# Causal attention with decay, then two expert layers, on one Trainium2 core: single fp32 score products, with new load order, start and last pair

## What is computed

```
scores = q @ k.T / sqrt(64);  cum = cumsum(log(clip(f, 1e-4, 1)))
attn   = softmax(where(j > i, -1e9, scores + cum[i] - cum[j]))
x      = (attn @ v), heads side by side: [1152, 512]
logits = x @ w_gate; expert = argmax; gate = its softmax probability
expert layer: relu(x @ w1[e]) @ w2[e], at most 288 rows an expert, times gate
dense layer:  h = x @ w_in; g = h if h >= 1, 0 if h <= -1, else (h+1)^2/4; out = g @ w_out
```

## Time and profile before

| | |
|---|---|
| median of 3 runs | 605.24 us (604.88 to 606.43) |
| the profiled execution | 605.88 us |
| its span, first to last instruction | 604.0 us |
| TensorE busy | 574.3 us (95%) |
| weight loads | 511.4 us (85%) |
| VectorE busy | 334.3 us (55%) |
| ScalarE busy | 286.5 us (47%) |
| GpSimd busy | 62.7 us (10%) |
| mean granted TensorE clock | 0.990 |

### The profile page before, as it was taken

How to read it: one execution, slowest core, us unless ns; L and a number is a source line. 1 busy time by engine, 2 the same in 40 slices (tenths; PEclk the granted TensorE clock), 3 DMA queues, 4 the chain that set the end, 5 groups by cost and what they waited for, 6 DMA issues and landing times.

```text
span 604.0 us, 9717 instructions
## 1 busy us (share of the span) xinstructions
PE 574.3 (95%) x3774; PEld 511.4 (85%) x3774; DVE 334.3 (55%) x657; ACT 286.5 (47%) x570; POOL 62.7 (10%) x75
## 2 busy tenths in 40 slices
PE   7869999999999999999999999989999999999993
PEld 3658888878448999999999999989999999999992
DVE  3748888875703545658456584786443543453432
ACT  3647777774303444736446364575333333333330
POOL 8301111110250500000000000000000200010001
PEclk9979999999999999999999999999999999999998
DMA  6984755520154056254562645633000100000001
GB/s 135 288 187 117 186 121 119 150 71 0 43 179 166 25 186 209 74 206 148 195 212 76 208 145 173 240 106 105 1 0 1 53 0 2 1 18 36 0 1 52
DMA packets 52973, 63.95 MB, mean 106 GB/s; under 512 B 31136, under 2 KB 31136, under 8 KB 52928
## 3 DMA queue, kind: packets, MB, share of 16 engines
q1 hardware_dynamic: 50960, 58.56, 32.0%
q0 software_dynamic: 1968, 4.77, 2.2%
HBM read 58.55 MB, written 4.77 MB: 105 GB/s over the span
## 4 chain that ended last, share of the span: by engine, by line
PE 81%; DVE 5%; SPq 4%; issue 3%; DMA 2%; POOL 2%; ACT 2%; DVEq 0%; ACTq 0%
PE ps L652 11%; PE ps L653 11%; PE ps L654 11%; PE ps L726 5%; PE ps L727 5%; PE ps L728 5%; PE ps L709 5%; PE ps L711 5%; PE ps L710 5%; PE ps L535 4%; PE ps L497 3%; PE ps L516 2%; PE ps L550 2%; POOL x_scratch L423 1%; SPq L313 1%
## 5 line engine op out<-in xcount | busy, mean ns | idle before, releaser
L276 DVE TENSOR_TENSOR slot<-stage,slot 128x1024 fp32r<-128x1024 f32 x80 | 95.4, 1221 | 20.7 <-ACT slot L269 20.7
L269 ACT ACTIVATE slot<-stage 128x1024 fp32r<-128x1024 f32 x80 | 81.4, 1052 | 4.6 <-DMA stage<-in_moe_w_in_dram 2.6
L872 ACT ACTIVATE act_t<-ps,half 128x384 f32<-128x384 f32 x48 | 27.9, 582 | 115.2 <-PE ps L711 115.2
L1138 DVE SCALAR_TENSOR_TENSOR act_t<-act_t 128x384 f32<-128x384 f32 x48 | 26.8, 558 | 99.1 <-ACT act_t L872 99.1
L652 PE MATMUL ps<-xe,slot 128*128 128x288 f32 x256 | 75.8, 296 | 0.3 <-DVE xe L1090 0.3
L653 PE MATMUL ps<-xe,slot 128*128 128x288 f32 x256 | 75.6, 295 | 0.0
L653 PE MATMUL ps<-hid,slot 128*128 128x288 f32 x256 | 75.6, 295 | 0.0
L654 PE MATMUL ps<-xe,slot 128*128 128x288 f32 x256 | 75.3, 294 | 0.0
L654 PE MATMUL ps<-hid,slot 128*128 128x288 f32 x256 | 75.3, 294 | 0.0
L652 PE MATMUL ps<-hid,slot 128*128 128x288 f32 x256 | 75.2, 294 | 0.0
L847 ACT ACTIVATE hid<-ps 128x288 fp32r<-128x288 f32 x64 | 26.5, 415 | 99.6 <-PE ps L654 98.7
(11 more groups left out here) (147 smaller groups left out, 1073.0 us busy)
## 6 DMA issues: line engine op xcount, KB each, us to landing
stage<-in_moe_w_dram SPq DMA_DIRECT2D x32, 1024.0 KB, 5.2
cb<-c_scratch SPq DMA_DIRECT2D x16, 288.0 KB, 3.6
x_sorted<-x_scratch SPq DMA_DIRECT2D x9, 258.0 KB, 4.8
cb<-c_scratch SPq DMA_DIRECT2D x16, 144.0 KB, 4.3
q_nat<-in_q_dram SPq DMA_DIRECT2D x16, 128.0 KB, 3.6
k_nat<-in_k_dram SPq DMA_DIRECT2D x16, 128.0 KB, 2.6
v_nat<-in_v_dram SPq DMA_DIRECT2D x16, 128.0 KB, 4.1
stage<-in_moe_w_in_dram SPq DMA_DIRECT2D x2, 1024.0 KB, 6.1
```

The lines of the kernel that those rows point to most:

```text
L269: nc.scalar.activation(s[:, 0, at], stages[n_buf][:, at], ACT.Copy).then_inc(w_hi, 1)
L276: nc.vector.tensor_tensor(s[:, 1, at], stages[stage_of(g)[0]][:, at], s[:, 0, at].bitcast(F32), ALU.subtract).then_inc(w_lo, 1)
```

## The change

- **Scores.** `q_t` and `k_t` hold one fp32 value; `qk_low` and the low parts are gone. `score` makes one fp32 product a head and tile where there were three fp32r ones.
- **Loads.** The first pair's keys, the decay inputs of its two heads and of all heads are issued by ScalarE. SyncE loads pairs 0, 1 and 2 and v of pair 0 before it waits for the decay sums; a pair's q and k are loaded two pairs ahead, pair 3 between weight chunks 0 and 1.
- **Decay sums.** Those of pair 0 are made on all partitions at once (spread load of f, logarithm, two scans), without the way through DRAM. The scan for the other heads comes after the first row maxima. `fl` lies in `xl`.
- **Weight parts.** High parts of the six halves at steps 6, 11, ... 31, low parts at 11, 16, ... 36, after the splitting of the probabilities.
- **128-row forms.** `ot` has 640 columns, the last 64 zero, so that the last tile's product with the router's weights has the full form; a matrix `shift` does the same for the row sums.
- **Start.** q and k of pair 0 are transposed into two banks (6 and 2) without a wait between.
- **Last pair.** The second product with v is cut into the tiles that need only the low parts up to the last but one (banks 0 and 1) and the last tile (bank 6). The logits of the earlier heads are summed ahead of time (`lg`), those of the last two are added.

```diff
+        q_t = sb("q_t", [P, 2, QT], F32, att)
+        k_t = sb("k_t", [P, 2, S], F32, att)
...
+        ot = sb("ot", [P, 2, NT * P], F32, att)
...
+        fl = xl[0:BH].rearrange("p h t c -> p (h t c)")[:, 0:3 * S].rearrange("p (r s) -> p r s", r=3)
...
-        EARLY = {n: (i // 2, i % 2) for i, n in enumerate([9, 14, 19, 24, 29, 34])}
+        EARLY_HI = {NT * (i + 1) + 1: (i // 2, i % 2) for i in range(6)}
+        EARLY_LO = {NT * (i + 2) + 1: (i // 2, i % 2) for i in range(6)}
...
-            load_pair(0)
-            sp.wait_ge(f_steps, 3)
-            sp.dma_start(c_dram[:, :], fl[:, 0, :]).then_inc(c_out, 16)
-            sp.wait_ge(c_out, 16)
-
...
+                if p >= 1:
+                    load_keys(sp, p)
+
+            def load_decay(p):
                 if p >= 2:
                     sp.wait_ge(maxed, UNITS * (p - 1))
-                    sp.wait_ge(v_lo, p - 1)
-                for hh in range(2):
-                    sp.dma_start(cb[:, p % 2, hh, :], c_dram[2 * p + hh:2 * p + hh + 1, :].partition_broadcast(P)
-                                 ).then_inc(c_in[p % 2], 16)
+                sp.dma_start(cb[:, p % 2, 0:2, :], c_dram[2 * p:2 * p + 2, :].partition_broadcast(P)).then_inc(c_in[p % 2], 16)
                 for hh in range(2):
                     sp.dma_start(cb[64 * hh:64 * hh + 64, p % 2, 2, :],
                                  c_dram[2 * p + hh:2 * p + hh + 1, :].partition_broadcast(64)).then_inc(c_in[p % 2], 16)
-                if p == 0:
...
+            def load_v(p):
+                b, h = divmod(2 * p, HEADS)
+                if p >= 2:
+                    sp.wait_ge(v_lo, p - 1)
...
-            load_decay_and_v(0)
-            load_decay_and_v(1)
+            load_pair(0)
+            load_pair(1)
+            load_v(0)
+            load_pair(2)
+            sp.wait_ge(f_steps, 3)
+            sp.dma_start(c_dram[:, :], fl[:, 0, :]).then_inc(c_out, 16)
+            load_v(1)
+            sp.wait_ge(c_out, 16)
+            load_decay(1)
             load_chunk(sp, 0)
+            load_pair(3)
             load_chunk(sp, 1)
             load_chunk(sp, 2)
             for p in range(2, PAIRS):
-                load_pair(p)
-                load_decay_and_v(p)
+                load_decay(p)
+                load_v(p)
+                if p + 2 < PAIRS:
+                    load_pair(p + 2)
                 if p == 4:
                     load_chunk(sp, 3)
...
+        def qk_bank(p, j):
+
+            return 2 if p == 0 and j == 1 else 6
...
             def score(n):
                 p, t = divmod(n, NT)
                 if t == 0:
-                    pe.wait_ge(qk_lo, 2 * p + 2)
+                    pe.wait_ge(qk_sb, 2 * p + 2)
                 if n >= 1:
                     pe.wait_ge(maxed, units_to(n - 1))
                 qs = slice(Q0[t], Q0[t] + P)
-                parts = ((0, 0), (1, 0), (0, 1))
                 if t < LAST:
-                    for i, (a, b) in enumerate(parts):
-                        for hd in range(2):
-                            r = slice(64 * hd, 64 * hd + 64)
-                            mm(bank(hd, W[t]), q_t[r, p % 2, a, qs], k_t[r, p % 2, b, 0:W[t]], start=(i == 0), stop=False)
+                    for hd in range(2):
+                        r = slice(64 * hd, 64 * hd + 64)
+                        mm(bank(hd, W[t]), q_t[r, p % 2, qs], k_t[r, p % 2, 0:W[t]], start=True, stop=False)
                     for hd in range(2):
                         last = mm(bank(hd, P, Q0[t]), ident_b[:], mask_b[:], start=False, stop=True)
                 else:
-                    for i, (a, b) in enumerate(parts):
-                        mm(bank(0), q_t[:, p % 2, a, qs], k_t[:, p % 2, b, 0:Q0[t]], start=(i == 0), stop=(i == 2))
-                        mm(bank(1, D), q_t[:, p % 2, a, qs], k_t[:, p % 2, b, Q0[t]:S], start=(i == 0), stop=False)
+                    mm(bank(0), q_t[:, p % 2, qs], k_t[:, p % 2, 0:Q0[t]], start=True, stop=True)
+                    mm(bank(1, D), q_t[:, p % 2, qs], k_t[:, p % 2, Q0[t]:S], start=True, stop=False)
                     last = mm(bank(1, D), ident_b[:], mask4_b[:], start=False, stop=True)
                 last.then_inc(scores, 1)
...
+            def output_tile(p, hd, t, to):
+
+                return mm(to, ot[:, hd, P * t:P * t + P], rg[:, (2 * p + hd) % HEADS, :], start=True, stop=True)
+
             def output(p, hd, b):
 
                 if p == 0 and hd == 0:
-                    pe.wait_ge(wg_in, 16 * 2 * HEADS)
+                    pe.wait_ge(wg_in, 32)
                     pe.wait_ge(consts, 1)
                 if hd == 0:
                     pe.wait_ge(exped, UNITS * (p + 1))
-                    mm(bank(b, 1, 448, 64), ident[:, 64:128], rowsum[:, p % 2, 0, LAST:NT], start=True, stop=True).then_inc(sum_ps, 1)
+                    mm(bank(b, 1, 448), shift[:], rowsum[:, p % 2, 0, LAST:NT], start=True, stop=True).then_inc(sum_ps, 1)
                 pe.wait_ge(o1_sb, 2 * p + hd + 1)
                 pe.wait_ge(o2_sb, 2 * p + hd + 1)
                 for t in range(NT):
-                    last = mm(bank(b, XC, XC * t, QN[t]), ot[:, hd, Q0[t]:W[t]], rg[:, (2 * p + hd) % HEADS, :], start=True, stop=True)
+                    last = output_tile(p, hd, t, bank(b, XC, XC * t))
                 last.then_inc(ox_ps, 1)
...
-            spin(6, 2)
-            pe.wait_ge(qk_lo, 1)
             transposed(0, 1)
-            spin(6, 2)
+            spin(8, 4)
             score(0)
...
+            pe.wait_ge(pt_lo, UNITS * PAIRS - 1)
+            pe.wait_ge(maxed, UNITS * PAIRS)
+            times_v_full_tiles(0, 0)
+            times_v_full_tiles(1, 1)
+            pe.wait_ge(exped, UNITS * PAIRS)
+            mm(bank(2, 1, 448), shift[:], rowsum[:, end % 2, 0, LAST:NT], start=True, stop=True).then_inc(sum_ps, 1)
+            for hd in range(2):
+                pe.wait_ge(o1_sb, 2 * end + hd + 1)
+                for t in range(2):
+                    output_tile(end, hd, t, bank(5 + 2 * hd, XC, XC * t))
+            pe.wait_ge(pt_lo, UNITS * PAIRS)
             pe.wait_ge(xl_sb, 2 * end)
-            times_v_second(end, 1, 6)
-            spin(4, 0)
-            pe.wait_ge(o1_sb, 2 * end + 2)
-            output(end, 0, 7)
-            output(end, 1, 6)
+            for hd in range(2):
+                times_v_last_tile(hd, 6, D * hd)
+            for hd in range(2):
+                pe.wait_ge(o2_sb, 2 * end + hd + 1)
+                for t in range(2, LAST):
+                    last = output_tile(end, hd, t, bank(5 + 2 * hd, XC, XC * t))
+                last.then_inc(ox_ps, 1)
+            pe.wait_ge(o_last, 1)
+            pe.wait_ge(r_inv, 3 * PAIRS)
+            for hd in range(2):
+                last = output_tile(end, hd, LAST, bank(2, XC, XC * hd))
+            last.then_inc(ox_last, 1)
...
+            act.dma_start(cb[:, 0, 0:2, :], f[0, 0:2, :].partition_broadcast(P)).then_inc(f0_in, 16)
+            load_keys(act, 0)
+            act.dma_start(fl[:, 0, :], f.rearrange("b h s -> (b h) s")).then_inc(f_in, 16)
+            act.wait_ge(f0_min, 1)
+            A.activation(ot[:, :, 0:S], cb[:, 0, 0:2, :], ACT.Ln).then_inc(f0_log, 1)
+            act.wait_ge(f_steps, 2)
...
+                if n in EARLY_HI:
+                    cut_hi(*EARLY_HI[n])
...
+            dve.wait_ge(f0_in, 16)
+            V.tensor_scalar(cb[:, 0, 0:2, :], cb[:, 0, 0:2, :], 1.0e-4, 1.0, ALU.max, ALU.min).then_inc(f0_min, 1)
             dve.wait_ge(f_in, 16)
             V.tensor_scalar(fl[:, 0, :], fl[:, 0, :], 1.0e-4, 1.0, ALU.max, ALU.min).then_inc(f_steps, 1)
-            V.memset(fl[:, 2, :], 1.0).then_inc(f_steps, 1)
-            dve.wait_ge(f_log, 1)
             dve.wait_ge(f_steps, 2)
-            V.tensor_tensor_scan(fl[:, 0, :], fl[:, 2, :], fl[:, 1, :], 0.0, ALU.mult, ALU.add).then_inc(f_steps, 1)
+            dve.wait_ge(f0_log, 1)
+            for hd in range(2):
+                V.tensor_tensor_scan(cb[:, 0, hd, :], ones, ot[:, hd, 0:S], 0.0, ALU.mult, ALU.add).then_inc(f0_sum, 1)
...
-            def qk_low(p, j):
-                dve.wait_ge(qk_hi, 2 * p + j + 1)
-                if j == 0:
-                    V.scalar_tensor_tensor(out=q_t[:, p % 2, 1], in0=bank(6, QT), scalar=-float(D) ** -0.5,
-                                           in1=q_t[:, p % 2, 0].bitcast(F32), op0=ALU.mult, op1=ALU.subtract).then_inc(qk_lo, 1)
-                else:
-                    V.tensor_tensor(k_t[:, p % 2, 1], bank(6, S), k_t[:, p % 2, 0].bitcast(F32), ALU.subtract).then_inc(qk_lo, 1)
-
...
+            dve.wait_ge(f_log, 1)
+            V.tensor_tensor_scan(fl[:, 0, :], ones[0:BH], fl[:, 1, :], 0.0, ALU.mult, ALU.add).then_inc(f_steps, 1)
...
+                if n in EARLY_LO:
+                    cut_lo(*EARLY_LO[n])
+                if n == 32:
+                    V.tensor_reduce(lg[:, 0:NT, :], xl[:, 0:HEADS, :, D:XC].rearrange("p h t e -> p t e h"), AX_X, ALU.add
```

(37 more changed lines are left out.)

120 lines of the change are left out of this document (57 added, 63 removed).

## The result

The changed kernel takes 588.51 us (median of 4 runs, 588.12 to 589.55); the kernel before, measured beside it, 605.06 (604.66 to 606.43). The ratio is 0.9725, with a 95% interval of 0.9705 to 0.9745: 16.5 us faster. The forecast was 595.0 with a range of 587 to 604, so the range held the time, near its low end, and rival A had the size. The profiled execution took 588.54 us, 17.34 less than that of before.

What follows compares the result with a forecast made beforehand. TensorE was taken as nearly full in all but the first slices. From the profiled 605.88: +2.8 (later pairs), -6.4 (stall), -3.7 (start), -3.0 (last pair) gave 595.6; the median, 0.64 lower, 595.0 us; range 587 to 604.

Steps and rivals of the forecast that it cites:

- rival A: Half-row fp32 score products: both heads overlap fully, 1.05 us a pair less than forecast, 587 us; chance 0.15.
- Score products: TensorE's score groups: one fp32 product a head instead of three fp32r ones adds 1.55 us a pair.
- three slots: Score group's four records: head 0's first, its second beside head 1's first, head 1's second; 2 passes each, 6N columns.
- 4N: Columns a score group streams with both heads fully overlapped, N being the tile's columns; +0.5 us a pair.
- k-low wait: TensorE's wait for VectorE's low part of k goes when qk_low is dropped: -0.15 us a pair.
- Weight cuts: VectorE's low cut moved from ahead of the 256-column maxima: -0.57 us a pair, -1.11 in the last.
- 128-row forms: Output and row-sum products of the last tile avoid switching to the 64-column form: -0.3 us a pair.
- Stall: Pair 0 to pair 1: loading pair 2 ahead of the weight chunks removes stall and slow clock; -6.4 us net.
- Start: Up to pair 0's last-tile scores: first scores at 10.4 instead of 13.09, last-tile scores at 19.5 instead of 23.18; -3.7 us.
- Last pair: Last scores to first maximum over the logits: full tiles start earlier, maximum at 151.9 instead of 154.87; -3.0 us.
- Rival C: SyncE's queue: pair 2's loads delay pair 1's decay, VectorE waits up to 4 us; 599 us, chance 0.1.

## Why the prediction was right, and where it was not

The direction and the range held: the sum was 595.6 for the profiled execution, 7.1 us above what it took. The range held by luck. The largest term, the cost of the score products, was wrong and made the forecast too slow; the start, also wrong, made it too fast by 2.6 us. With the start as predicted and all else the same the time would have been about 586, below the range. By stretches of the table the miss is 7.8 us in the six periods, 0.7 in pair 1, 0.2 in the last pair and 0.95 behind it, less 2.6 at the start. By its steps:

- **Score products, +1.55 us a pair: failed, +0.40.** The 4 passes a product were right (0.21 us for each 128 columns; the last tile, without halves, went from 1.08 to 1.14 us). The step that failed is the assumption that "the second record of head 0 needs the same rows as the first and waits for it", and so three slots. The two heads' first records start together and their second ones too; the group costs 4N columns, as rival A had it, and at 128 columns it is 0.06 us cheaper than before where I took 0.09 more. That is 1.15 us a pair, about 9 over 8 pairs: more than the whole miss. The rule of the Trainium skill (TensorEngine Tiling (Array Packing), section Key Properties), that tiles work independently, agrees with this case: both heads take 1.06 us at 512 columns, one alone 1.05. Its other rule, that true fp32 takes 4 passes (FP8 and Floating Point Precision, section TensorE Precision Notes), agrees with the 0.21 us for each 128 columns; that the reduced form takes one is read from the rows of before (0.17 us for three products of 128 columns). It spoke against this part, and in TensorE's own time rightly: 0.37 us a pair.
- **k-low wait, -0.15:** right, -0.23. **Weight cuts, -0.57:** right in cause. Not foreseen: with two waits in one VectorE stream, taking one away leaves a part at the next place (the two transposes, 0.14 to 0.36, and 0.14 again with the cuts undone). Undoing the cuts alone costs 0.75.
- **128-row forms, -0.3:** right in cause, 0.40 by the run.
- **Stall, -6.4:** right, 7.14 in the trace, though the sum had 1.15 us too much for pair 1's score products in it. Undone alone it costs 9.24, with a stall of 6.84 us and the slow clock around it.
- **Start, -3.7: failed, -1.08.** The step was "first scores at 10.4". I costed what the engines do and left out in what order ScalarE's stream stands: two logarithms and a table load ahead of the copies, and the second logarithm waiting for f behind the keys. The small load of f, which that logarithm needs, landed at 9.21, and I had given it no place in the chain: with it ahead of the keys the first scores come at 11.61. I also took the clock there for granted, which cost nothing until that was mended.
- **Last pair, -3.0:** right, -3.19. More than half of it is the early start of the full tiles (1.89 us by the run). Behind it are 0.95 us that I costed at nothing; they lie behind the last store's issue, and their cause stays open.

Rival C did not happen: from 14 to 45 us VectorE waits for no decay rows. Undoing one part at a time costs 9.4 us (loads), 4.9 (cuts), 1.4 to 2.65 (forms, in the time and to the one-hot product) and 4.7 (single product, only at the ends), more together than the 16.5 of the change, so the parts are not additive, or some of these costs are slow stretches of the clock that came with the run and not with the edit, as at the end of the run with late low cuts.

## What to carry to other kernels

Before an operation is made cheaper, look at who waits behind it: the single product costs TensorE more and frees VectorE, and nets to nothing in a middle pair, while the place of the weight cuts is worth 5 us and the order of the loads 9 us. Read a start by each engine's order of instructions and each queue's order of loads; the operation that waits longest holds all that is queued behind it, needed or not. Of full fp32 products on half the rows, two heads cost as much as one, if nothing that uses all rows stands between them.

## What the runs showed that I had not expected

The granted clock falls in stretches of some microseconds that are not tied to a long stall. It fell to the lower level after 2.4 to 2.6 us without work ahead of the first transposes in some executions and not after 2.60 and 2.90 in two others; and in the run with 24 early fillers and 4 later ones it fell to 0.50 at 134 us, in products of 64 and 72 columns that leave no gap, where the changed kernel ran the same products at 1.00. The five executions of that kernel took 586.3, 587.96, 587.98, 589.2 and 589.54 us at mean clocks of 0.996, 0.994, 0.994, 0.991 and 0.991: the time follows the clock. A fall at the end of attention is in four of the twelve experiments' traces, among them the heads kept apart and the three products with late cuts, and costs 1.5 to 3.2 us on the way to the one-hot product. No run shows what brings it about. Differences between versions of under 2 us are therefore not resolved by these medians: f ahead of the keys is 1.36 us earlier at pair 0 in the trace, but its ratio overlaps that of the changed kernel, and no version here is shown to beat it.
